# GpSimd rounds the first up-weight tiles during the attention prelude, and three steps of the prelude change places

## The reference

```python
# 1. windowed attention: 2 batches, 8 heads, 576 positions, head size 64, window 64
scores = q @ k.T / 8
scores = where((rel >= 0) & (rel < 64), scores, -1e9)     # rel = query position - key position
attn = exp(scores - max(scores)); attn = attn / (attn.sum(-1) + 1e-9)
x = (attn @ v)  -> 1152 tokens x 512
# 2. MLP: w_in 512 x 2048, w_out 2048 x 512
h = x @ w_in
x = (maximum(h, 0) + log1p(exp(-abs(h)))) @ w_out
# 3. four gated experts: w1 512 x 1024, w2 1024 x 512
out = sum_e p[:, e:e+1] * (maximum(x @ w1[e], 0) @ w2[e])
```

## Time and profile before

| | us |
|---|---|
| median of 3 runs | 633.42 |
| the profiled execution, whole | 633.28 |
| its span in the trace | 631.5 |
| PE busy | 621.8 (98%) |
| DVE busy | 388.5 (62%) |
| ACT busy | 275.9 (44%) |
| POOL busy | 86.7 (14%) |

### The profile page before, as it was taken

The page is one execution under the profiler, slowest core; times in us unless marked ns, Lnnn a source line. Parts: engine busy times, 40 slices in busy tenths (PEclk is TensorE's granted clock), DMA queues, the critical chain, the costliest instruction groups (busy, mean ns, idle before and its releaser), DMA issues.

```text
span 631.5 us, 10128 instructions
## 1 busy us (share of the span) xinstructions
PE 621.8 (98%) x3880; PEld 578.4 (92%) x3880; DVE 388.5 (62%) x867; ACT 275.9 (44%) x634; POOL 86.7 (14%) x84
## 2 busy tenths in 40 slices
PE   7999999999999999999999999999999999999997
PEld 6789999999999999998998998988988988988986
DVE  5987665577645588887267277276276376376342
ACT  5887755556544465552342342332332432432410
POOL 1453333323332332000000000000000000000000
PEclk9999999999999999999999999999999999999999
DMA  8915130023200010023102103003003003000012
GB/s 329 366 42 199 70 134 1 28 106 134 67 2 0 2 34 31 3 67 101 35 0 101 34 1 102 33 1 109 26 1 120 15 1 131 4 0 1 2 51 100
DMA packets 11584, 40.78 MB, mean 65 GB/s; under 512 B 2320, under 2 KB 2320, under 8 KB 10256
## 3 DMA queue, kind: packets, MB, share of 16 engines
q1 hardware_dynamic: 11536, 40.13, 18.1%
HBM read 37.77 MB, written 2.36 MB: 64 GB/s over the span
## 4 chain that ended last, share of the span: by engine, by line
PE 95%; DMA 1%; DVE 1%; ACT 1%; POOL 1%; issue 0%; SPq 0%; DVEq 0%
PE banks L1062 31%; PE banks L1049 28%; PE banks L1018 16%; PE banks L998 16%; PE banks L959 2%; DMA raw_b<-in_w_out 1%; PE banks L985 1%; PE banks L972 1%; PE banks L1068 1%; ACT prob L462 1%; DVE prob L660 0%; POOL wa_lo L427 0%; DVE prob L646 0%; DVE wb_lo L634 0%; POOL sp_c L423 0%
## 5 line engine op out<-in xcount | busy, mean ns | idle before, releaser
L1062 PE MATMUL banks<-wb_hi,ehid_hi 128*128 128x512 f32 x288 | 112.1, 389 | 0.0
L1062 PE MATMUL banks<-wb_lo,ehid_hi 128*128 128x512 f32 x288 | 112.1, 389 | 0.0
L1062 PE MATMUL banks<-wb_hi,ehid_lo 128*128 128x512 f32 x288 | 112.0, 389 | 0.0
L423 POOL TENSOR_TENSOR sp_c<-sp_e,sp_c 128x384 f32<-128x384 f32 x48 | 64.2, 1338 | 134.9 <-DVE sp_c L676 134.9
L810 DVE SCALAR_TENSOR_TENSOR part<-banks,gate,part 128x512 f32<-128x512 f32 x63 | 47.3, 751 | 55.9 <-PE banks L1062 55.9
L1049 PE MATMUL banks<-T_lo,aop_hi 128*128 128x288 f32 x256 | 75.6, 295 | 0.0
L1049 PE MATMUL banks<-T_hi,aop_lo 128*128 128x288 f32 x256 | 75.6, 295 | 0.0
L1049 PE MATMUL banks<-T_hi,aop_hi 128*128 128x288 f32 x256 | 75.3, 294 | 0.0
L998 PE MATMUL banks<-xy_hi,wa_hi 128*128 128x384 f32 x192 | 66.3, 345 | 0.0
L1018 PE MATMUL banks<-hid_hi,wb_hi 128*128 128x384 f32 x192 | 65.8, 343 | 0.1
L1062 PEld LDWEIGHTS banks<-wb_hi,ehid_lo 128*128 128x128 f32 x288 | 54.1, 188 | 11.2
(11 more groups left out here) (98 smaller groups left out, 1233.6 us busy)
## 6 DMA issues: line engine op xcount, KB each, us to landing
unit_in<-in_units SPq DMA_DIRECT2D x8, 1024.0 KB, 7.7
raw_a<-in_w SPq DMA_DIRECT2D x16, 512.0 KB, 3.3
raw_b<-in_w SPq DMA_DIRECT2D x16, 512.0 KB, 3.3
raw_a<-in_w_in SPq DMA_DIRECT2D x8, 512.0 KB, 5.2
raw_b<-in_w_out SPq DMA_DIRECT2D x8, 512.0 KB, 4.2
out_dram<-part SPq DMA_DIRECT2D x9, 256.0 KB, 2.0
part<-in_units SPq DMA_DIRECT2D x2, 1024.0 KB, 12.4
unit_in<-in_units SPq DMA_DIRECT2D x2, 384.0 KB, 6.5
```

The source lines that it names most:

```text
L423: pool.tensor_tensor(sp_c[:, s, :], sp_e[:, s, :], sp_c[:, s, :], ALU.subtract).then_inc(lost_done, 1)
L1062: m = pe.matmul(TOKEN_BANKS[T], ehid[x][:, i, P * T:P * T + P], wb[a][:, f, :], start=(i == 0 and j == 0), stop=(i == 3 and j == 2))
```

## The change

Four things change, all in the first 35 us of the program:

1. The rounding of up-weight tiles 0 to 4 moves from DVE to GpSimd (`up_high`). GpSimd now goes through a tile at a time, copy and then the two low halves, as soon as the raw tile has landed; its waits on `norm_done` are gone.
2. The first down-weight tile is rounded by ACT, behind the last exponential of the prelude, and its low part is made by GpSimd in two halves (`down_low_half`), ahead of up-weight tile 4.
3. Unit 0's three exponentials each wait for their own maximum (`first_maxima`) in place of all three.
4. On DVE `masked_scores(2)` goes ahead of `row_inverse(1)` and `normalise_first(1)`. Unit 10 is normalised by DVE in step 0 in place of GpSimd, ahead of the `activation` of that step.

```diff
-        FIRST_SPLIT = {3: 0, 4: 1, 5: 2, 6: 3, 9: 4}
+        N_FIRST = 5
 # GpSimd
-            for i in range(len(FIRST_SPLIT) - 1):
-                pool.wait_ge(wa_hi, i + 1)
-                up_low_half(i // 2, i % 2)
-            for i, unit in zip(range(len(FIRST_SPLIT) - 1, 2 * len(FIRST_SPLIT)), (7, 8, 8, 9, 9, 9)):
-                pool.wait_ge(norm_done, unit + 1)
-                if i == 8:
-                    pool.wait_ge(wa_hi, 5)
-                up_low_half(i // 2, i % 2)
+            def down_low_half(half):
+                cols = slice(DM // 2 * half, DM // 2 * half + DM // 2)
+                low = pool.tensor_tensor(wb[1][:, 0, cols], raw_b[:, 0, 0, cols], f32(wb[0][:, 0, cols]), ALU.subtract)
+                if half == 1:
+                    low.then_inc(wb_lo, 1)
+
+            def up_high(f):
+                pool.wait_ge(raw_a_in[f // 2 % 2], 16 * (f // 4 + 1))
+                pool.tensor_copy(wa[0][:, f, :, :],
+                                 raw_a[:, f // 2 % 2, :, P * (f % 2):P * (f % 2) + P]).then_inc(wa_hi, 1)
+                pool.wait_ge(wa_hi, f + 1)
+
+            for f in range(N_FIRST):
+                if f == N_FIRST - 1:
+                    pool.wait_ge(wb_hi, 1)
+                    down_low_half(0)
+                    down_low_half(1)
+                up_high(f)
+                up_low_half(f, 0)
+                up_low_half(f, 1)
             for k in range(STEPS):
                 lost(k // FT, k % FT)
-                if k + SCORED < N_UNITS:
+                if 0 < k < N_UNITS - SCORED:
                     normalise(k + SCORED)
 # ScalarE, softmax_exp(u)
-                act.wait_ge(negmax_done, u + 1)
                 for w in range(3):
+                    if u == 0 and w < 2:
+                        act.wait_ge(first_maxima, w + 1)
+                    elif w == 0 or u == 0:
+                        act.wait_ge(negmax_done, u + 1)
 # ScalarE, behind the prelude's rounds
+            split_down(0, 0)
 # VectorE
             row_inverse(0)
             normalise_first(0)
+            masked_scores(2)
             row_inverse(1)
             normalise_first(1)
-            masked_scores(2)
...
-                if j == SCORED - 1:
-                    down_high(0)
-                    split_down(0, 0)
                 row_inverse(j)
                 normalise_first(j)
-                if j in FIRST_SPLIT:
-                    up_high(FIRST_SPLIT[j])
...
                     row_inverse(k + SCORED)
+                    if k == 0:
+                        normalise_first(SCORED)
```

More of the change, by code:

```diff
@@ L249, in two_stage_mlp_after_window_attention @@
         negmax_done = sem("negmax_done")
+        first_maxima = sem("first_maxima")
         exp_done = sem("exp_done")
@@ L648, in masked_scores @@
                                                  negmax[:, u % 3, w:w + 1])
+                    if u == 0 and w < 2:
+                        e.then_inc(first_maxima, 1)
                 e.then_inc(negmax_done, 1)
@@ L814, in _ @@
             dve.wait_ge(consts, N_CONSTS)
[L815 to L824, removed]
             masked_scores(0)
```

## The result

| | before | after |
|---|---|---|
| median, us | 633.62 (13 runs) | 635.05 (13 runs, 634.43 to 636.17) |
| the profiled execution, whole / its span | 633.28 / 631.5 | 635.25 / 633.5 |

The ratio is 1.0022, with an interval of 1.0015 to 1.0029: the change costs 1.4 us. I had forecast 2.2. In the profiled executions the spans lie 2.0 apart.

A forecast was written before the change was run, and what follows sets the result against it. DVE was taken to bound the prelude, with a full PE queue behind it. Waits of 3.56 us less 0.54 and 1.0 gave 2.0, and 0.1 to 0.2 more made 2.2: 635.6 us, range 634.8 to 636.8.

The forecast's parts named there:

- Where the time is set: End of the prelude: PE's queue is full from up product 4 on, so its 2.2 us later start moves the span.
- GpSimd's copy: Rounding an up-weight tile on GpSimd: a 128x512 copy was put at 0.63 us.
- the slow copy: Rival: GpSimd's copy takes 1.25 us, so up product 4 comes 4.8 later, 638.2 us; chance 0.12.
- The two engines shut each other out: Prelude: a GpSimd instruction blocks DVE's double-rate ones, multiplications included, until 0.13 us before its end.
- The first rival: GpSimd does not stop DVE's multiplications: up product 4 comes 1.4 us earlier, 632.0 us; chance 0.17.
- The walk through units 3 to 5: DVE's normalising beside GpSimd's tile work: instruction by instruction, 3.56 us of waiting in all.
- the turn between each two instructions: Units 3 to 5: a GpSimd instruction already asking goes in between two DVE instructions, as at the low part at 37.24.
- The second rival: DVE keeps the ports through the three multiplications, so each unit loses one wait: 0.7 us later, 634.1 us; chance 0.13.
- The gain at the head: Before unit 6's transposes: 0.54 us from unit 4's earlier scores and 1.0 from three roundings off DVE, against the waits.
- The second place: Units 9 and 10: waits beside down-weight halves, tile 4 and `lost` 0, mostly offset by other edits; 0.1 to 0.2 us net.
- the mark of the forecast: Start of up product 4, at 43.81 us before, expected at 46.0, 2.2 later.
- The sum: Whole program: span 631.5 + 2.2 = 633.7 us, 635.5 for the profiled execution, 635.6 as median.

The follow-up runs named there:

- e4: The changed kernel with DVE's normalising multiplications also writing a sum nothing reads, so that they run at one element a cycle: 633.41 us.
- e9: The changed kernel run once more, unaltered, for a second trace: 634.59 us, ratio 1.0019 to the kernel before.
- e10: The changed kernel with GpSimd's copy of each next up-weight tile ahead of the halves of the current one: 635.16 us.
- e1: The kernel before with only unit 0's early exponentials and unit 2's maxima ahead of unit 1's inverse: 633.21 us.
- e3: The changed kernel with the rounding of up-weight tiles 0 to 4 back on DVE and GpSimd's halves waiting as before: 633.50 us.
- e12: The changed kernel with e4's multiplications, GpSimd's tile 4 and `lost` 0 ahead of the down-weight halves, and the third attention-input group in two DMAs: 633.12 us.

## Why the prediction was right in kind and too large in size

**Where the time is set: right.** T11 and up product 4 move with the span in every trace. PE's queue behind them has no new gaps.

**GpSimd's copy: right.** 0.60 to 0.62 us against 0.63; the slow copy (638.2) is out.

**The two engines shut each other out, the multiplications included: right, and shown by e4.** Before the run this rested on a deduction from three durations, with no row of the two side by side. The first rival (not stopped) is refuted: the multiplications do wait. Its price was wrong too, for even where they don't (e4) the time is 633.41 and not 632.0. In part that is e4's slower form, 0.07 us each. In part it is the addition of unit 10, which that rival left free and which lost 0.77 to `lost` 0 in e4.

**The walk through units 3 to 5: this term was 0.4 too large.** I had 3.56 us, the traces show 3.14 and 3.13. The step that failed is the turn between each two instructions. I had taken it from the one case in the earlier trace rows, where GpSimd was already asking, and carried it to a place where GpSimd first waits 0.08 us for its own semaphore; in unit 4 DVE slips a second multiplication in there. By unit the walk had 1.27, 1.68 and 0.61, and the first trace shows 1.12, 1.00 and 1.02: unit 4 lost one wait less, and a part of that was lost again, because DVE came to unit 5 sooner (in e9 its first multiplication is asked for at 20.22, in the walk at about 21.0) and met one half more. With the pause taken out (e10) no second multiplication slips in. Each single wait was also slightly off: a multiplication ends 0.08 us behind GpSimd (GpSimd's half at 14.67 + 1.42 = 16.09, the second multiplication of unit 3 at 14.92 + 1.25 = 16.17, by the rows below), where 0.28 from a start 0.13 early, 0.15, had been counted. DVE's timeline of the changed kernel, cut behind the second multiplication:

```profile
14.92 1.25 DVE L679 TENSOR_SCALAR prob<-prob,rinv 128x128 f32<-128x128 f32 x2
```

The second rival (one wait per unit, the second and third multiplication free) is out in all three units: of those two, both waited in unit 3, the third in unit 4, the second in unit 5, and both in every unit of e10.

**The gain at the head: right in size.** T6 of e9 is 23.67 = 22.09 + 3.13 - 1.55, and 1.55 is what I had set against the waits (0.54 and 1.0). The first part is seen by itself: DVE takes up scores 4 at 12.76 in e9, 0.58 earlier than before.

```profile
12.76 0.29 DVE L663 CUSTOM_DVE_ANT_0 prob<-banks,mask 128x128 f32<-128x128 f32 x1 [0.21 <-PE banks L964]
```

e1 and e3 still round on DVE and can show this part alone: T6 comes 0.52 and 0.59 earlier, but T11 only 0.26 and 0.23. In e4, where the roundings are gone as well, T6 is 0.45 earlier; its multiplications take some 0.2 us more in each round. So a gain at the head isn't all left at T11 when DVE is no longer late.

**The second place: 0.5 too large.** From T6 to the transposes of unit 10 I expected a little more than before, 11.8; before it is 11.65, after (both traces) 11.21. To up product 4, the mark of the forecast, it is 21.72 before and 21.37 in e9, 0.35 less where I had 0.15 more. At units 9 and 10 DVE lost 0.97 + 0.48 = 1.45 us, seen in groups of 1.65 and 1.16 where 0.68 is usual. I had counted some 2.5, among them 0.6 for tile 4 beside the first softplus step, where DVE lost nothing, and 0.77 for `lost` 0 ahead of the inverse of unit 10. That one did not happen either: GpSimd began `lost` 0 at 34.19, and DVE was there first, at 34.10. In e4 and e12 the two came the other way round, and the addition lost 0.77 and 0.63. An order that hangs on 0.1 us can't be forecast by a walk with errors of 0.4.

**The sum.** 2.2 - 0.4 - 0.5 = 1.3, and e9 shows 1.2. The first trace shows 2.0, because a landing 0.8 late came on top: that it is so near the forecast 2.2 is luck. Before, DVE took up scores 4 only at 13.34, 0.5 us after it could have; now, with DVE behind through unit 5, a late landing counts in full.

## What to carry to other kernels

Work that moves from VectorE to GpSimd isn't gone from VectorE's time if VectorE's own instructions there run at two elements a cycle, or are tiny ones of that kind: each can lose most of a GpSimd instruction, and an addition of 0.16 us lost as much (0.46) as a multiplication (0.48). So look first at the durations of what will run beside the moved work. If the two must overlap, a form of the VectorE operation at one element a cycle, 0.06 to 0.07 us slower each, can be the faster one (633.41 against 635.05). That was seen for an instruction with one tensor as its input; the subtraction of two tensors in the earlier trace rows took 1.32 and not 0.68 beside GpSimd, although it runs at one element a cycle.

## What the runs showed of the hardware

- A VectorE instruction that is shut out is on record with its start before the wait, so it looks long (up to 0.78 us and not 0.28) and has no idle time and no releaser. In the chain the wait of the first is "issue". Only the mean of its group and the other engine's rows give it away.
- GpSimd hardly suffers: its pairs of halves for tiles 0 to 3 took 1.41 to 1.47 us in the traces with these tiles in a row, while VectorE lost 2.8 to 3.6 us in the same stretch (in e4, where only the small additions can wait, 0.1).
- Who goes next when both are asking depends on 0.08 us: with GpSimd's next instruction ready, VectorE gets one multiplication through (0.68 us apart); where GpSimd first waits for its own result, it gets two.
- The landing of a 1 MB transfer moved by 0.8 us between two executions of the same kernel (8.69 and 9.50 us on the chain), and what was queued behind it moved along.
